# An attention and two-MLP kernel: x2 transposed by VectorE in squares of 32 and placed by DMA, where TensorE and two ScalarE copies did it

## The chip, the cores and the metric

One core of one Trainium2 chip. The time is the device time of one execution in microseconds (us), and the median of several executions is given. Around the profiled execution's span (first to last instruction) lie some 2 us that its time also counts.

## The reference, cut to what matters

```python
def _attn_ref(q, k, v, n_sink, window):            # 2 x 8 heads x 768 x 64
    scores = scale * np.matmul(q, k.transpose(0, 1, 3, 2))
    keep = is_sink | in_window                      # 4 sinks, a window of 128
    a = softmax(np.where(keep, scores, -1e9))
    return np.matmul(a, v)

x = attention, laid out as 1536 tokens x 512
h = x @ w_in                                        # 512 -> 1024
ln = layernorm(h * softmax(h)) * g_ln
x2 = ln @ w_out                                     # 1024 -> 512
g = np.maximum(x2 @ w2_in, 0.0) ** 2                # 512 -> 2048
out = g @ w2_out                                    # 2048 -> 512
```

## The kernel before, in words

The 1536 tokens are worked as NT = 12 tiles of 128. Tile numbers run from 0 to 11. Products are in fp32r: each operand is split into a rounded part (`_hi`) and a rest (`_lo`), and each product is three matmuls.

**Stage A** makes attention, h, the gated layer norm and x2 for one tile after another, as a pipeline that is written out by hand for each engine. `step(t)` (one function of this name on TensorE, ScalarE and VectorE) does at the same time: the values and `hidden` (h) of tile n = t + 1, the transposes of the normalised hidden row `u` and the second projection (`project`, into `x2_ps`) of tile t, and the scores and softmax of tile t + 2. `first_step` and `second_step` are steps 0 and 1; then come steps 2 to 10, the last without scores. Each engine runs its list in order, and semaphores tie the lists together, so where an instruction stands in a list decides what waits behind it.

**x2 before the change.** The matmuls of `project(t, ...)` (L1240) leave x2 of tile t as 128 tokens x 512 in the PSUM bank `x2_ps`, which is the bank `w1_ps` (rows of the trace say `w_ps`). Stage B needs it transposed, with the 512 features on the partitions. So

- ScalarE's `copy_x2` (L622) copies it to the SBUF tile `x2` (rows say `x`), first thing in the next step;
- TensorE's `transpose_x2(t - 1)` (L1268) transposes four blocks of 128x128 into `o_ps`, between `transpose_p(t + 2, 0)` and `transpose_p(t + 2, 1)`, near the end of the step;
- ScalarE's `copy_x2T` (L626) copies `o_ps` into columns t*128 to t*128+127 of `x2T`, a [128, 4, 1536] tile.

`transpose_ln(t)` (L1230) may not overwrite `w1_ps` until `copy_x2(t - 1)` is done, and `values(n, 0)` may not write `o_ps` until `copy_x2T` of tile n - 3 is done.

**VectorE in a step** normalises `u` (`normalize_hidden`, L883, which waits for GpSimd's `rstd`, L444), splits xT and lnT, merges scores and takes the row maxima of tile t + 2 (L827, L839), normalises probabilities in two groups (`normalize_p`, L899 to L904), splits the next K and Q (`split_k` L888, `split_q` L893), takes the maximum of h (`hidden_max`, L844, two halves), and then gates and does the statistics of tile n (`gate_and_norm`, L854 to L871).

**SyncE's queue** issues nearly all DMAs in order. Its loop over n waits for `q_split` and loads Q (L319), waits for `k_split` and loads K (L326), waits for `pv_done` and loads V of tile n - 1 (L331), and for n = 4 to 7 loads a quarter of `w2in` (L378). After the loop it loads the last V, waits for h of tile 11 (`h_done`, 2 * NT) and issues the eight loads of `w2out` (L383).

**Stage B** takes 3 blocks of 512 tokens. `round_x2T(blk)` on ScalarE (L755) and `split_x2T(blk)` on VectorE (L1054) make the two parts of x2T, all four tiles of a block at once; `hidden2` (L1405) and `project2` (L1417) are the products, with `chain` on ScalarE and VectorE in between. The first `hidden2` calls of block 0 are laced with the end of tile 11:

```python
            hidden2(0, 0)
            transpose_x2(NT - 2)
            hidden2(0, 1, 0, 2)
            transpose_ln(NT - 1)
            hidden2(0, 1, 2, 3)
            project(NT - 1, 0, 12).then_inc(wo_half_read, 1)
            project(NT - 1, 12, 24)
            hidden2(0, 1, 3, 4)
            transpose_x2(NT - 1)
```

`project2` writes four banks, one of which is `w1_ps`, so x2 of tile 11 must be out of it before block 0 goes on.

Of the kernel before, what the change touches and what calls it, by code (L numbers as in the profile page):

```python
# [49 lines left out]
BLK = BANK  # L50
NB = T // BLK
# [79 lines left out]
def attention_moe_program(nc, qT, kT, v, w_in, w_out, g_ln, w2_in, w2_out, out):  # L131
# [6 lines left out]
    with ctx:  # L138
# [141 lines left out]
        x2_done, x2T_done = sem("x2_done"), sem("x2T_done")  # L280
# [4 lines left out]
        lnT_split, xT_split, x2T_copied = sem("lnT_split"), sem("xT_split"), sem("x2T_copied")  # L285
# [4 lines left out]
        lnT_rounded, xT_rounded, x2_copied = sem("lnT_rounded"), sem("xT_rounded"), sem("x2_copied")  # L290
# [21 lines left out]
        @block.sync  # L312
        def _(sp):
            def load_q(n):
                if since(n, 3):
                    sp.wait_ge(q_split, n - 2)
                for half in range(2):
                    rows, heads = half_heads(half)
                    sp.dma_start(q_raw[rows, :, :], qT[n, :, heads, :]).then_inc(q_loaded, 16)  # L319

            def load_k(n):
                if since(n, 3):
                    sp.wait_ge(k_split, n - 1)
                for half in range(2):
                    rows, heads = half_heads(half)
                    sp.dma_start(k_raw[rows, :, :], kT[n, :, heads, :]).then_inc(k_loaded, 16)  # L326

            def load_v(n):
                if since(n, 2):
                    sp.wait_ge(pv_done, GROUPS * n)  # L330
                sp.dma_start(V[:, n % 2, :], v[n]).then_inc(v_loaded[n % 2], 16)  # L331

            def load_w_in(c):
                sp.dma_start(w_raw[:, c, :], w_in[c * P:(c + 1) * P, :]).then_inc(w_loaded[c], 16)

            def load_w_out(c):
                sp.dma_start(wo_raw[:, c * C1 // 2:(c + 1) * C1 // 2, :],
                             w_out[c * F1 // 2:(c + 1) * F1 // 2, :].rearrange("(k p) m -> p k m", p=P)
                             ).then_inc(wo_loaded[c], 16)

            def load_k01(n):
                for half in range(2):
                    rows, heads = half_heads(half)
                    sp.dma_start(k01[rows, n, :, :], kT[n, :, heads, :]).then_inc(k01_loaded[n], 16)

            def load_v_sink(b):
                sp.dma_start(v_sink_raw[0:SKS, b, :],
                             v[b * TPB, 0:N_SINK, :].unsqueeze(0).to_broadcast([SPLITS * H, N_SINK, DM])
                             ).then_inc(v_sink_loaded[b], 16)

            load_k01(0)
            load_w_in(0)
            load_w_in(1)
            load_v(0)
            load_k01(1)
            for half in range(2):
                load_q01(sp, 1, half)
            load_w_in(2)
            load_v_sink(0)
            load_w_in(3)  # L360
            load_k(2)
            load_q(2)
            load_v(1)
            load_w_out(0)
            load_w_out(1)
            load_v_sink(1)
            for n in range(3, NT):
                load_q(n)
                load_k(n)
                load_v(n - 1)  # L370
                if n == 4:
                    sp.wait_ge(w_split, MC - 1)
                    sp.wait_ge(w_split_pool, 4)
                    sp.wait_ge(wo_split, len(WO_DVE))
                    sp.wait_ge(wo_split_pool, len(WO_POOL))
                if n in range(4, 4 + MC):
                    c = n - 4
                    sp.dma_start(w2in[:, c, :], w2_in[c * P:(c + 1) * P, :]).then_inc(w2in_loaded, 16)  # L378
            load_v(NT - 1)
            sp.wait_ge(h_done, 2 * NT)  # L380
            sp.wait_ge(h_done, 2 * NT)
            for c in range(C2 // 2):
                sp.dma_start(w2out[:, 2 * c:2 * c + 2, :],  # L383
                             w2_out[2 * c * P:(2 * c + 2) * P, :].rearrange("(c p) m -> p c m", p=P)
                             ).then_inc(w2out_loaded[c], 16)
            with sp.Fori(0, NB) as blk:
                for i in range(TB):

                    sp.wait_ge((y_copied_act, y_copied_dve)[i % 2], TB // 2 * blk + (i // 2 + 1))
                    sp.dma_start(out[bass.ds(blk * BLK + i * P, P), :], y[i]).then_inc(y_stored, 16)  # L390
            sp.wait_ge(y_stored, 16 * TB * NB)

# [156 lines left out]
        def _(act):  # L549
# [70 lines left out]
            def copy_x2(t):  # L620
                act.wait_ge(x2_done, t + 1)
                nc.scalar.copy(x2[:, :], x2_ps[:, :]).then_inc(x2_copied, 1)  # L622

            def copy_x2T(t):
                act.wait_ge(x2T_done, t + 1)
                nc.scalar.activation(x2T[:, :, bass.ts(t, P)], o_ps[:, :].rearrange("p (c q) -> p c q", q=P),  # L626
                                     ACT.Copy).then_inc(x2T_copied, 1)

# [8 lines left out]
            def step(t, nxt=True):  # L637
# [3 lines left out]
                copy_x2(t - 1)  # L641
# [16 lines left out]
            def finish(t):  # L658
# [8 lines left out]
                copy_x2T(t - 1)  # L667
# [26 lines left out]
            def second_step():  # L694
# [5 lines left out]
                copy_x2(0)  # L700
# [51 lines left out]
            def round_x2T(blk):  # L752
                cols = slice(blk * BLK, (blk + 1) * BLK)
                act.wait_ge(x2T_copied, TB * (blk + 1))
# [10 lines left out]
            copy_x2T(NT - 3)  # L765
            hidden_exp(NT - 1)
            copy_x2(NT - 2)
            copy_x2T(NT - 2)
# [18 lines left out]
            copy_x2(NT - 1)  # L787
            chain(1, 1)
            copy_x2T(NT - 1)
# [17 lines left out]
        def _(dve):  # L807
# [110 lines left out]

            def split_v_sink(b):
# [12 lines left out]
            def step(t):  # L932

                n = t + 1
                normalize_hidden(t)
# [5 lines left out]
                row_max(t + 2, 0)  # L941
                merge(t + 2, 2)
# [3 lines left out]
                if t + 3 < NT:  # L946
                    split_k(t + 3)
                    split_q(t + 3)
                hidden_max(n, 0)
                hidden_max(n, 1)  # L950
                hidden_max_all(n)
                normalize_p(t + 2, 1)
# [30 lines left out]
            def second_step():  # L983
# [11 lines left out]
                row_max(3, 0)  # L995
                merge(3, 2)
# [65 lines left out]

            normalize_hidden(NT - 2)
# [7 lines left out]
            gate_and_norm(NT - 1)  # L1071
            normalize_hidden(NT - 1)
# [20 lines left out]
            split_w2out(0)  # L1093
            chain(1, 1)
# [17 lines left out]
        def _(pe):  # L1112
# [41 lines left out]
            def values(n, g):  # L1154

                if g == 0:
                    pe.wait_ge(v_loaded[n % 2], 16 * (n // 2) + 16)
                    if since(n, 3):
                        pe.wait_ge(x2T_copied, n - 2)
# [64 lines left out]
            def transpose_ln(t):  # L1224
                if t:
                    pe.wait_ge(x2_copied, t)
# [36 lines left out]
            def transpose_x2(t):  # L1263
                pe.wait_ge(x2_copied, t + 1)
                if t >= NT - 2:
                    pe.wait_ge(x2T_copied, t)
                for c in range(MC):
                    done = nc.tensor.transpose(o_ps[:, c * P:(c + 1) * P], x2[:, c * P:(c + 1) * P], ident[:, :])  # L1268
                done.then_inc(x2T_done, 1)

# [4 lines left out]
            def step(t, nxt=True):  # L1275
# [23 lines left out]
                transpose_x2(t - 1)  # L1299
# [31 lines left out]
            def second_step():  # L1331
# [19 lines left out]
                transpose_x2(0)  # L1351
# [84 lines left out]
            transpose_x2(NT - 2)  # L1436
# [6 lines left out]
            transpose_x2(NT - 1)  # L1443
# [36 lines left out]
```

## Time and profile before

| | before |
|---|---|
| median of 3 runs | 504.12 us (503.33 to 504.96) |
| the profiled execution's own time | 503.94 us |
| its span | 502.1 us |
| TensorE (PE) busy | 489.4 us, 97% |
| weight loads (PEld) busy | 398.0 us, 79% |
| VectorE (DVE) busy | 279.6 us, 56% |
| ScalarE (ACT) busy | 212.7 us, 42% |
| GpSimd (POOL) busy | 99.0 us, 20% |
| chain that ended last, by engine | PE 86%, DVE 11%, ACT 1%, POOL 1% |
| granted TensorE clock | 0.999 of full |

Busy shares are averages over a stage A of some 240 us and a stage B of some 260 us. A matmul's row is longer than its place in the pipeline: the chain of waits gives the pace (0.23 us a matmul of 512 columns), the single rows give 0.39 us.

### The profile page before, as it was taken

The page shows a single profiled execution, that of the slowest core. Times are in us where ns is not written, and L with a number is a line of the kernel's source. Part 1 is how long each engine was busy: PE and PEld are TensorE (multiplying, and loading weights), DVE is VectorE, ACT ScalarE, POOL GpSimd, SP SyncE. Part 2 cuts the span into 40 slices and gives each one's busy share as a digit, 9 for nine tenths or more (in the row PEclk, how much of TensorE's full clock was granted, in tenths as well). Part 3 has the DMA queues.
Part 4 walks back from the last instruction along what each step waited for, and adds up shares of the span by engine and source line. Part 5 has one row for each costly group of instructions (what it writes and reads, how often), then busy time and mean ns, then how long its engine had stood idle before and what let it go on. Part 6 is the DMA issues. An engine that isn't in the chain of part 4 may idle for free.

```text
span 502.1 us, 7242 instructions
## 1 busy us (share of the span) xinstructions
PE 489.4 (97%) x2692; PEld 398.0 (79%) x2692; DVE 279.6 (56%) x501; ACT 212.7 (42%) x556; POOL 99.0 (20%) x138
## 2 busy tenths in 40 slices
PE   8989899999999999999999999999999999999997
PEld 6667778888788888878877888888888888888885
DVE  4999798777878878756696433332222232232232
ACT  4667556656666665624543322421211232221121
POOL 2555051020022112264994000000000000000000
PEclk9999999999999999999999999999999999999999
DMA  8921241241112100008000000020000002000002
GB/s 254 282 66 46 103 144 48 106 147 44 52 35 63 44 22 22 1 4 332 1 0 2 0 0 1 1 84 0 0 0 0 0 0 84 1 0 0 1 0 84
DMA packets 12069, 26.05 MB, mean 52 GB/s; under 512 B 1608, under 2 KB 1608, under 8 KB 11528
## 3 DMA queue, kind: packets, MB, share of 16 engines
q1 hardware_dynamic: 11736, 25.40, 15.6%
q8 instruction: 18, 0.29, 0.2%
q10 hardware_dynamic: 304, 0.27, 0.2%
q14 instruction: 11, 0.09, 0.1%
HBM read 22.52 MB, written 3.15 MB: 51 GB/s over the span
## 4 chain that ended last, share of the span: by engine, by line
PE 86%; DVE 11%; ACT 1%; POOL 1%; issue 1%; DVEq 0%; POOLq 0%; ACTq 0%
PE score_ps L1405 25%; PE h_ps L1417 12%; PE w_ps L1240 11%; PE h_ps L1202 11%; PE wt_ps L1417 6%; PE w_ps L1417 6%; PE o_ps L1172 3%; PE score_ps L1142 2%; PE wt_ps L1150 2%; PE wt_ps L1142 1%; PE h_ps L1230 1%; DVE prob L904 1%; PE o_ps L1268 1%; PE w_ps L1273 1%; PE o_ps L1189 1%; DVE w2out_lo L1059 1%
## 5 line engine op out<-in xcount | busy, mean ns | idle before, releaser
L1405 PE MATMUL score_ps<-x2T_hi,w2in_hi 128*128 (+1 forms) x192 | 74.9, 390 | 0.0
L1405 PE MATMUL score_ps<-x2T_hi,w2in_lo 128*128 (+1 forms) x192 | 74.7, 389 | 0.0
L1405 PE MATMUL score_ps<-x2T_lo,w2in_hi 128*128 (+1 forms) x192 | 74.7, 389 | 0.0
L1076 DVE TENSOR_TENSOR e<-e 128x512 f32<-128x512 f32 x24 | 18.5, 772 | 81.7 <-ACT e L772 81.7
L1076 DVE TENSOR_TENSOR sq<-relu 128x512 f32<-128x512 f32 x24 | 17.5, 728 | 80.5 <-ACT relu L772 80.5
L772 ACT ACTIVATE relu<-score_ps 128x512 f32<-128x512 f32 x24 | 14.3, 598 | 92.1 <-PE score_ps L1405 92.1
L772 ACT ACTIVATE e<-score_ps 128x512 f32<-128x512 f32 x24 | 14.4, 599 | 87.4 <-PE score_ps L1405 87.3
L1405 PEld LDWEIGHTS score_ps<-x2T_hi,w2in_hi 128*128 128x128 f32 x192 | 36.1, 188 | 7.5
L1405 PEld LDWEIGHTS score_ps<-x2T_hi,w2in_lo 128*128 128x128 f32 x192 | 36.0, 188 | 7.4
L1405 PEld LDWEIGHTS score_ps<-x2T_lo,w2in_hi 128*128 128x128 f32 x192 | 36.0, 188 | 7.4
L582 ACT ACTIVATE prob<-sm,nbias 128x132 f32<-128x132 f32 (+1 forms) x96 | 37.8, 396 | 0.5
L1240 PE MATMUL w_ps<-wo_hi,lnT_hi 128*128 128x512 f32 x88 | 35.5, 404 | 2.3 <-DVE lnT_lo L911 2.2
L1202 PE MATMUL h_ps<-w_hi,xT_hi 128*128 128x512 f32 x88 | 35.5, 404 | 0.7 <-DVE xT_lo L916 0.7
L1240 PE MATMUL w_ps<-wo_lo,lnT_hi 128*128 128x512 f32 x88 | 35.3, 401 | 0.0
L1202 PE MATMUL h_ps<-w_hi,xT_lo 128*128 128x512 f32 x88 | 34.5, 392 | 0.0
L1240 PE MATMUL w_ps<-wo_hi,lnT_lo 128*128 128x512 f32 x88 | 34.4, 390 | 0.0
L1202 PE MATMUL h_ps<-w_lo,xT_hi 128*128 128x512 f32 x88 | 34.3, 390 | 0.0
L544 POOL TENSOR_TENSOR w2in_lo<-w2in,w2in_hi 128x512 fp32r<-128x512 f32 x16 | 25.5, 1597 | 1.3
L601 ACT ACTIVATE e<-h_ps,nhmax 128x512 f32<-128x512 f32 x24 | 16.3, 684 | 18.9 <-DVE nhmax L849 18.8
L425 POOL CAST p_sink<-prob 128x64 fp32r<-128x64 f32 x10 | 2.4, 237 | 110.8 <-DVE prob L904 99.8
L1240 PEld LDWEIGHTS w_ps<-wo_hi,lnT_hi 128*128 128x128 f32 x88 | 16.5, 188 | 7.2 <-DVE lnT_lo L911 3.1
L1202 PEld LDWEIGHTS h_ps<-w_hi,xT_hi 128*128 128x128 f32 x88 | 16.5, 188 | 5.3 <-issue 1.2
(180 smaller groups left out, 1133.5 us busy)
## 6 DMA issues: line engine op xcount, KB each, us to landing
w2in<-w_in SPq DMA_DIRECT2D x4, 1024.0 KB, 4.9
w2out<-w_out SPq DMA_DIRECT2D x8, 512.0 KB, 7.4
V<-v SPq DMA_DIRECT2D x12, 256.0 KB, 2.6
k_raw<-kT SPq DMA_DIRECT2D x20, 132.0 KB, 2.8
q_raw<-qT SPq DMA_DIRECT2D x20, 128.0 KB, 2.8
w2in<-w_in SPq DMA_DIRECT2D x4, 512.0 KB, 6.5
w2in<-w_out SPq DMA_DIRECT2D x2, 1024.0 KB, 11.6
out<-u SPq DMA_DIRECT2D x6, 256.0 KB, 2.0
```

Source lines behind the costliest of these rows:

```text
L544: nc.gpsimd.tensor_tensor(w2in_lo[:, :, fs], w2in[:, :, fs], w2in_hi[:, :, fs].bitcast(F32), ALU.subtract).then_inc(w2in_split, 1)
L582: nc.scalar.activation(prob[:, h, seen(n)], sm[:, h, seen(n)], ACT.Exp, bias=nbias[:, h:h + 1], scale=SCALE, accum_out=psum_row[:, h:h + 1 ...
L601: nc.scalar.activation(e[:, cols], h_ps[:, cols], ACT.Exp, bias=nhmax[:, :], scale=1.0, accum_out=hsum[:, half:half + 1]).then_inc(h_exped, 1)
L772: nc.scalar.activation(relu[f % 2], h2_ps[f % 2], ACT.Relu).then_inc(relu_ready, 1)
L1076: nc.vector.tensor_tensor(sq[f % 2], relu[f % 2], relu[f % 2], ALU.mult).then_inc(sq_ready, 1)
L1142: done = mm(score_banks(n, p)[:, j, cols], qs[rows], ks[rows], start=(n < 2 or i == 0), stop=(n < 2 or i == len(products) - 1))
L1150: last = nc.tensor.transpose(pT_ps[g][:, j * P:(j + 1) * P], prob[:, g * HG + j, main(n)], ident[:, :])
L1172: last = mm(o_ps[rows, cols], V[:, slot, h * D:(h + 1) * D], pT[:, g, j * P:(j + 1) * P], start=(g == 0 and part == 0 and i < 2), stop=(al ...
L1202: done = mm(h_ps[:, cols], xs[:, c, :], ws[:, c, cols], start=(c == 0 and k == 0), stop=(c == MC - 1 and k == 2))
L1240: done = mm(x2_ps[:, :], ls[:, k, :], ws[:, k, :], start=(k == 0 and i == 0), stop=(k == C1 - 1 and i == 2))
L1405: done = mm(h2_ps[f % 2], ws[:, c, fs], xs[:, c, bass.ts(blk, BLK)], start=(c == 0 and i == 0), stop=(c == MC - 1 and i == 2))
L1417: done = mm(y_ps[q], gs[f % 2][:, qs], ws[:, f, :], start=(f == 0 and i == 0), stop=(f == C2 - 1 and i == 2))
```

## The change

VectorE transposes `x2_ps` into `x2` in one instruction, each square of 32x32 in its place. A square then has the right inside and the wrong place: the 16 pairs (token quarter i, feature quarter r) are carried to x2T by 16 DMAs a tile, each of 32 partitions x 4 chunks x 32 elements (128 bytes a run). `transpose_x2`, `copy_x2` and `copy_x2T` and their waits go. On VectorE `split_q` and `normalize_p(t + 2, 1)` also move forward.

```diff
+SQ = 32
+QUADS = P // SQ
+MOVES = 16 * QUADS * QUADS
...
+            def move_x2(t):
+
+                sp.wait_ge(x2_squared, t + 1)
+                squares = x2[:, :].rearrange("p (c r b) -> p c r b", r=QUADS, b=SQ)
+                for i in range(QUADS):
+                    for r in range(QUADS):
+                        sp.dma_start(x2T[r * SQ:(r + 1) * SQ, :, t * P + i * SQ:t * P + (i + 1) * SQ],
+                                     squares[i * SQ:(i + 1) * SQ, :, r, :]).then_inc(x2T_moved[t // TB], 16)
...
             for n in range(3, NT):
+                if n >= 5:
+                    move_x2(n - 5)
                 load_q(n)
                 load_k(n)
                 load_v(n - 1)
...
+            move_x2(NT - 5)
             load_v(NT - 1)
-            sp.wait_ge(h_done, 2 * NT)
+            move_x2(NT - 4)
+            move_x2(NT - 3)
             sp.wait_ge(h_done, 2 * NT)
             for c in range(C2 // 2):
                 sp.dma_start(w2out[:, 2 * c:2 * c + 2, :],
                              w2_out[2 * c * P:(2 * c + 2) * P, :].rearrange("(c p) m -> p c m", p=P)
                              ).then_inc(w2out_loaded[c], 16)
+            move_x2(NT - 2)
+            move_x2(NT - 1)
...
-                copy_x2(t - 1)
...
-                copy_x2T(t - 1)
...
-                act.wait_ge(x2T_copied, TB * (blk + 1))
+                act.wait_ge(x2T_moved[blk], TB * MOVES)
...
-            copy_x2T(NT - 3)
             hidden_exp(NT - 1)
-            copy_x2(NT - 2)
-            copy_x2T(NT - 2)
...
+            def square_x2(t):
+
+                dve.wait_ge(x2_done, t + 1)
+                if t:
+                    dve.wait_ge(x2T_moved[(t - 1) // TB], (t - 1) % TB * MOVES + MOVES)
+                nc.vector.transpose(x2[:, :], x2_ps[:, :]).then_inc(x2_squared, 1)
...
             def step(t):
 
                 n = t + 1
+                square_x2(t - 1)
                 normalize_hidden(t)
...
                 row_max(t + 2, 0)
+                if t + 3 < NT:
+                    split_q(t + 3)
                 merge(t + 2, 2)
                 merge(t + 2, 3)
                 row_max(t + 2, 1)
                 normalize_p(t + 2, 0)
                 if t + 3 < NT:
                     split_k(t + 3)
-                    split_q(t + 3)
                 hidden_max(n, 0)
+                normalize_p(t + 2, 1)
                 hidden_max(n, 1)
                 hidden_max_all(n)
-                normalize_p(t + 2, 1)
                 gate_and_norm(n)
...
+            square_x2(NT - 2)
             normalize_hidden(NT - 1)
...
             chain(0, 0)
             split_w2out(0)
+            square_x2(NT - 1)
             chain(1, 1)
...
-                    if since(n, 3):
-                        pe.wait_ge(x2T_copied, n - 2)
...
                 if t:
-                    pe.wait_ge(x2_copied, t)
+                    pe.wait_ge(x2_squared, t)
...
-                transpose_x2(t - 1)
...
             hidden2(0, 1, 3, 4)
-            transpose_x2(NT - 1)
+            pe.wait_ge(x2_squared, NT)
```

In `second_step` the transpose of tile 0 stands after `row_max(3, 0)`, and that of tile 9 ahead of `normalize_hidden(NT - 2)`.

VectorE, from the row maximum of the first group to the gate in a middle step, before (`nmax` is the row maximum, `QL` the split of Q, `hmax` the two halves of the maximum of h, `prob` the normalised probabilities):

```order
L839 TENSOR_REDUCE nmax<-sm 128x4
L827 COPY_PREDICATED sm<-own_seen,score_ps 128x2x128
L827 COPY_PREDICATED sm<-own_seen,wt_ps 128x2x128
...
L904 TENSOR_TENSOR prob<-prob,rz 128x528
L888 TENSOR_TENSOR KL<-k_raw,KH 128x4x132
L893 TENSOR_TENSOR QL<-q_raw,QH 128x512
L844 TENSOR_REDUCE hmax<-h_ps 128x1 x2
L849 TENSOR_REDUCE nhmax<-hmax 128x1
L899 TENSOR_SCALAR z_eps<-psum_row 128x4
L901 RECIPROCAL rz<-z_eps 128x4
L904 TENSOR_TENSOR prob<-prob,rz 128x528
L854 TENSOR_TENSOR u<-h_ps,e 128x512
```

and now, with the start of the step ahead of it (line numbers of the changed kernel):

```order
L872 TENSOR_TENSOR var<-moments,hz_eps 128x1
L925 STREAM_TRANSPOSE x<-w_ps 128x512
L884 TENSOR_SCALAR u<-u,moments,rstd 128x512 x2
...
L840 TENSOR_REDUCE nmax<-sm 128x4
L894 TENSOR_TENSOR QL<-q_raw,QH 128x512
L828 COPY_PREDICATED sm<-own_seen,score_ps 128x2x128
...
L845 TENSOR_REDUCE hmax<-h_ps 128x1
L900 TENSOR_SCALAR z_eps<-psum_row 128x4
L902 RECIPROCAL rz<-z_eps 128x4
L905 TENSOR_TENSOR prob<-prob,rz 128x528
L845 TENSOR_REDUCE hmax<-h_ps 128x1
L850 TENSOR_REDUCE nhmax<-hmax 128x1
L855 TENSOR_TENSOR u<-h_ps,e 128x512
```

The transpose stands between the variance and the normalisation; QL moved ahead of the second pair of merges, and the second group of probabilities moved between the halves of the maximum of h.

SyncE's queue at the end of stage A, before:

```order
L319 DMA q_raw<-qT 64x512 x2
L326 DMA k_raw<-kT 64x528 x2
L331 DMA V<-v 128x512 x2
L383 DMA w2out<-w_out 128x2x512 x8
```

and now (L342 is the DMA of the moves):

```order
L342 DMA x2T<-x 32x4x32 x16
L322 DMA q_raw<-qT 64x512 x2
L329 DMA k_raw<-kT 64x528 x2
L334 DMA V<-v 128x512
L342 DMA x2T<-x 32x4x32 x16
L334 DMA V<-v 128x512
L342 DMA x2T<-x 32x4x32 x32
L399 DMA w2out<-w_out 128x2x512 x8
L342 DMA x2T<-x 32x4x32 x32
```

Sixteen moves stand ahead of each Q load from tile 5 on, 32 ahead of the w2out loads and 32 behind them.

## Rows read from the trace of the kernel before

**Rows 1.** Chain that ended last, a middle step: start us, us, what.

```profile
156.08 0.44 PE o_ps L1268 x4
...
161.40 0.24 PE w_ps L1230 x2
...
174.11 0.44 PE o_ps L1268 x4
...
175.09 1.83 PE w_ps L1240 x8
```

**Rows 2.** The same chain, second step.

```profile
63.62 1.21 DVE hmax L844 x2
```

**Rows 3.** Timeline of DVE, same middle step: start, us, instruction, [idle before].

```profile
158.94 0.48 DVE L871 TENSOR_TENSOR var<-moments,hz_eps 128x1 f32<-128x1 f32 x1
160.09 1.00 DVE L883 TENSOR_SCALAR u<-u,moments,rstd 128x512 f32<-128x512 f32 x2 [0.68 <-POOL rstd L444]
...
166.50 0.45 DVE L827 COPY_PREDICATED sm<-own_seen,score_ps 128x256 f32<-128x256 uint32 x1 [1.06 <-ACT sm L555]
...
171.67 0.69 DVE L844 TENSOR_REDUCE hmax<-h_ps 128x1 f32<-128x512 f32 x1 [0.46 <-PE h_ps L1202]
...
172.87 0.71 DVE L904 TENSOR_TENSOR prob<-prob,rz 128x528 f32<-128x528 f32 x1
```

**Rows 4.** One line's instructions, L1012: a DVE subtraction of 128x1024.

```profile
L1012 DVE TENSOR_TENSOR w_lo<-w2in,w_hi x3: 1218/1219/1626, 13.2 to 24.1; 128x1024 fp32r<-128x1024 f32 x3
```

**Rows 5.** Timeline of SP's queue: the middle step, then the w2out loads.

```profile
160.85 0.33 SPq L331 DMA_DIRECT2D V<-v  x1
170.64 1.10 SPq L319 DMA_DIRECT2D q_raw<-qT  x2
...
224.57 4.76 SPq L383 DMA_DIRECT2D w2out<-w_out  x8
```

**Rows 6.** One line's DMAs, L319 and L347: issue ns min/median/max, landing us.

```profile
L319 SPq DMA_DIRECT2D q_raw<-qT x20: 465/597/603, 9.5 to 171.1; - x20
...
DMA to landing us min/median/max: 2.5/2.8/8.5
```

```profile
L347 SPq DMA_DIRECT2D v_sink_raw<-v x2: 945/1226/1508, 6.8 to 12.4; - x2
```

**Rows 7.** Timeline of ACT: the middle step, then step 10.

```profile
159.43 0.63 ACT L573 ACTIVATE QH<-q_raw 128x512 fp32r<-128x512 f32 x1
```

```profile
226.99 0.60 ACT L626 ACTIVATE x2T<-o_ps 128x512 f32<-128x512 f32 x1 [8.12 <-PE o_ps L1268]
227.49 0.68 ACT L601 ACTIVATE e<-h_ps,nhmax 128x512 f32<-128x512 f32 x1
```

**Rows 8.** DMA queues: packets, MB, share of 16 engines; DMA issues with landing.

```profile
q1 hardware_dynamic: 11736, 25.40, 15.6%
...
q10 hardware_dynamic: 304, 0.27, 0.2%
...
out<-u SPq DMA_DIRECT2D x6, 256.0 KB, 2.0
...
x2T<-qT ACTq DMA_DIRECT2D x2, 128.0 KB, 4.0
...
g_col<-g_ln ACTq DMA_DIRECT2D x1, 4.0 KB, 5.5
```

**Rows 9.** Chain that ended last, end of stage A.

```profile
241.07 0.65 PE o_ps L1268 x4
241.72 0.69 PE wt_ps L1417 x3
```

**Rows 10.** Timeline of DVE, statistics of tile 11.

```profile
224.51 0.69 DVE L844 TENSOR_REDUCE hmax<-h_ps 128x1 f32<-128x512 f32 x1 [2.03 <-PE h_ps L1202]
...
231.52 0.16 DVE L871 TENSOR_TENSOR var<-moments,hz_eps 128x1 f32<-128x1 f32 x1
```

**Rows 11.** Busy time by stretch; the last two numbers are DMA share and GB/s.

```profile
236.00:238.00 2.00, 2.00 (x11) 1.65 (x10) 1.97 (x2) 0.29 (x1) 1.96 (x2) 1.00 0.77 299
```

More of the change, by code:

```diff
@@ L279, in attention_moe_program @@
         o_done, h_done, lnT_done = sem("o_done"), sem("h_done"), sem("lnT_done")
-        x2_done, x2T_done = sem("x2_done"), sem("x2T_done")
+        x2_done = sem("x2_done")
         maxed, biased, hmax_part, hmax_ready = sem("maxed"), sem("biased"), sem("hmax_part"), sem("hmax_ready")
@@ L284, in attention_moe_program @@
         z_ready, rz_ready, p_normed = sem("z_ready"), sem("rz_ready"), sem("p_normed")
-        lnT_split, xT_split, x2T_copied = sem("lnT_split"), sem("xT_split"), sem("x2T_copied")
+        lnT_split, xT_split, x2T_moved = sem("lnT_split"), sem("xT_split"), [sem(f"x2T_moved{b}") for b in range(NB)]
         w_rounded, w_rounded_act, w_split, wo_rounded, wo_split = sem("w_rounded"), sem("w_rounded_act"), sem("w_split"), sem("wo_rounded"), sem("wo_split")
@@ L289, in attention_moe_program @@
         exped, pT_copied, p_sinkT_copied, h_exped = sem("exped"), sem("pT_copied"), sem("p_sinkT_copied"), sem("h_exped")
-        lnT_rounded, xT_rounded, x2_copied = sem("lnT_rounded"), sem("xT_rounded"), sem("x2_copied")
+        lnT_rounded, xT_rounded, x2_squared = sem("lnT_rounded"), sem("xT_rounded"), sem("x2_squared")
         x2T_rounded, x2T_split = sem("x2T_rounded"), sem("x2T_split")
@@ L618, in round_xT @@
                                      ACT.Copy).then_inc(xT_rounded, 1)
[L620 to L627, printed above, removed]
             def round_w_out(first, last):
@@ L699, in second_step @@
                 round_q(4)
-                copy_x2(0)
                 bias(3, 0)
@@ L786, in _ @@
             round_w2out(0)
-            copy_x2(NT - 1)
             chain(1, 1)
-            copy_x2T(NT - 1)
             for f in range(1, C2):
@@ L995, in second_step @@
                 row_max(3, 0)
+                square_x2(0)
                 merge(3, 2)
@@ L1060, in split_w2out @@
                                         ALU.subtract).then_inc(w2out_split, 1)
+            square_x2(NT - 3)
             normalize_hidden(NT - 2)
@@ L1261, in project_0 @@
                     done.then_inc(x2_done, 1)
[L1263 to L1269, printed above, removed]
             def keep_warm(products):
@@ L1435, in _ @@
             hidden2(0, 0)
-            transpose_x2(NT - 2)
             hidden2(0, 1, 0, 2)
```

1 line of the change is left out of this document (removed).

## The prediction

> **What bounds the kernel now.** I read the page first: TensorE is busy 97% of the span, so only what shortens TensorE's list, or makes it wait, moves the time. Then the chain that ended last. In a middle step every piece of it is TensorE, one right behind the other; the reader should see that the four transposes of x2 stand in it with 0.44 us [rows 1], at 0.11 us each, because they are pipelined. From one set to the next is 174.11 - 156.08 = 18.0 us, the length of a step. In the second step the chain runs through VectorE instead [rows 2], so what TensorE saves there is worth nothing. Third, the timelines of VectorE, ScalarE and SP's queue, to see whether what is added fits in gaps, and last the end of stage A, where tile 11 is handed to stage B.
>
> **What is removed.** TensorE loses 12 sets of transposes. Tile 0's is off the chain: 0. Tiles 1 to 8, in steps 2 to 9: 8 x 0.44 = 3.52. Tile 9, in step 10, and tile 10, inside `hidden2`: 0.44 each. Tile 11's costs 0.65, since it waits for ScalarE's copy [rows 9]. Together 3.52 + 0.88 + 0.65 = 5.05 us. ScalarE's 24 copies (0.60 us each) stand ahead of work that waits for something else, so they are priced at nothing, with one exception: `copy_x2T(9)` holds `hidden_exp(11)` back. The second half of the maximum ends at 225.20 [rows 10] and a small reduction (about 0.2) follows, yet the exp starts at 227.49, behind a copy that waited for TensorE [rows 7]. So the statistics of tile 11 come 2.1 us earlier.
>
> **VectorE's transpose in a middle step.** No row shows this operation. VectorE's work on 512 columns out of PSUM takes 0.69 [rows 3]; an instruction of 1024 columns takes 1.22 [rows 4]. I take 0.70, one pass over as many columns, and keep 1.22 as the upper end. Below 0.69 I see no reason, and it would bring nothing, as the next lines show. It stands after the variance, which ends at 159.42, and ahead of the normalisation, which waits until 160.09 for GpSimd's rstd [rows 3]: 0.67 us idle that just about hold it. Its input, the end of `project`, is there at 158.9 (175.09 + 1.83 a step later shows the same place [rows 1]) and comes 0.44 earlier now. So the transpose ends at 160.16 and the first half of `u` at about 160.7, 0.1 later than before. TensorE asks for it at 161.40 [rows 1], now 0.44 earlier, 160.96. Slack 0.25: cost 0. With 1.22 us it would be 0.27 late, in each of 9 steps: 2.4 us.
>
> **The two moves on VectorE.** QL (0.68) goes into an idle 1.06 us before the third merge [rows 3]: 0. `normalize_p(t + 2, 1)`, 1.1 us, fills the 0.46 idle before the second half of `hmax` and the room that QL left; I place that half at 171.8 for 171.67, and the gate, which stood behind the same `normalize_p` until that ended at 173.58 [rows 3], no longer does. The chain to the variance keeps its time: 0. The probabilities come 1.7 us earlier, so TensorE can close the gap that the x2 transposes leave.
>
> **SP's queue in a middle step.** 16 DMAs of 16 KB a tile. Back to back, a Q load takes 0.60 us to issue [rows 6], the eight w2out loads 4.76 / 8 = 0.595 [rows 5], with four to eight times the bytes. The dearest issues are the v_sink loads, 0.945 and 1.508 [rows 6], whose two sides have different shapes (24 x 4 rows on 96 partitions). The moves have the same shape on both sides, so I take 0.60, near the many rows, and keep 0.33 (the V load, [rows 5]) and 1.51 as ends. The moves start behind the V load, 160.85 + 0.33 = 161.2, and end at 170.8; the Q load was issued at 170.64 [rows 5]. Nothing is late: it lands 2.8 us later [rows 6], and ScalarE's `round_q` comes at 159.43 + 17.57 = 177.0 [rows 7]. In numbers: the second Q load has landed 1.42 + 0.33 + 16c + 0.6 + 2.8 = 5.15 + 16c after the `round_q` before it, c being the issue cost; that must be under 17.57, so c may be 0.77. Next behind Q stand K and V with several us of slack. The wait of `square_x2(t)` for tile t - 1's moves is met 4 us ahead. Cost 0.
>
> **Packets.** A move is 128 runs of 128 bytes, 8 for each of 16 engines, and one semaphore write for each: 144 packets an engine and tile. Queue q1's mean packet takes 15.6% x 16 x 502.1 / 11736 = 107 ns at 2.2 KB [rows 8]: upper end, 15.4 us a tile. On ACT's queue q10 there are 304 packets in about 16 us: 128 of 2 KB, 128 of 32 bytes, 48 for semaphores; with the large ones at 107 ns the small ones are left 14 ns, and 36 ns if the rounded share is 0.25% [rows 8]. I take 14 to 36, 2.0 to 5.2 us a tile, less than the 9.6 us that issuing takes. The Trainium skill (DMA: Bandwidth & Descriptors, Specifications) says that a transfer under 512 bytes is a read-modify-write and misses line rate; it gives no price for 128 bytes, and no row here shows a read-modify-write; by it the sum would move towards the upper end, 512.7 (third rival below), where by the rows of q10 it stays at -2.5.
>
> **The end of stage A** is where a new wait appears. Times are those of before, less the 3.52 us gained by then. h of tile 11 is done at 224.5 - 3.5 = 221.0. SP has finished tile 9's moves at 220.3 (transpose done at 210.6, and 9.6 us), so the w2out loads go out at 221.0 to 225.8 and drain at about 234.3 (before, the stretch to 238 still moved 299 GB/s [rows 11]). The variance of tile 11 ends at 231.68 [rows 10] - 3.52 - 2.11 = 226.05, the transpose of tile 10 at 226.75, its moves are issued until 226.8 + 9.6 = 236.4 and land 2.0 us later (the shortest landing [rows 8]), at 238.4. Only then may VectorE transpose tile 11, though x2 is there at 236.0: done at 239.15. TensorE has nothing left from 241.07 - 4.40 = 236.67 [rows 9] and resumes at 239.2, where it resumed at 241.72 [rows 9]. So 2.5 us of the 5.05 are given back: -5.05 + 2.5 = -2.5 us. Behind the waiting transpose on VectorE stands `chain(1, 1)`, whose result TensorE wants only 5 us after it resumes. After that stage B is as before, earlier by 2.5.
>
> **The sum.** 503.94 (the profiled execution, 0.18 under the median) - 2.5 = 501.4 us.
>
> **Rivals.**
> - *The end gives all back.* With 53 ns a packet, behind w2out's drain at 234.3, tile 10 lands at 241.9, TensorE resumes at 242.7, +1.0: 505. The transpose at 1.22 us also ends here: -2.5 + 2.4 + 0.5, 504. For it: moves queue behind 4 MB in the same rings. Against: q10's small packets look cheap. 0.22.
> - *Slower: SP's queue becomes the bound of a step.* It decides at c = 0.77 for the steps and near 0.73 for the end. At 0.945 a step lasts 5.15 + 15.1 = 20.3, +2.7 for each of the 7 Q loads with moves ahead, 19 us; at the end tile 9's moves hold w2out and tile 10's hold TensorE, +9.3: 503.9 - 2.5 + 19 + 9.3 = 530. At 1.508 it would be 610. For it: the v_sink rows. Against: more than 60 issues at 0.6 or under. 0.17.
> - *Slower: the packets, or a fixed cost of each DMA.* At 107 ns, tile 10 lands at 249.7, TensorE resumes at 250.5, +8.8: 512.7, and Q loads land behind 15.4 us of packets and start to hold ScalarE. If DMAs did not overlap at all, 16 of the shortest landing, 2.0 [rows 8], would take 32 us against a step of 17.6, and `square_x2` would wait 14 us in each of 9 steps: 630. Against: two Q loads issued 0.6 apart each land 2.8 after their own issue [rows 6]. 0.11. The Trainium skill (DMA: Bandwidth & Descriptors, Anatomy of one DMA) fits 2.0 us + bytes / 436e3 to one DMA on the software path; added up that is an estimate of 33 us a tile, as in this rival; overlapped, it is only the landing. The trace speaks for overlap.
> - *Better: no wait at the end* (issue at 0.33 to 0.4 once the rings are free, quick packets): -5.0, 498.9. 0.10, within "faster".
>
> That the change does less than it says I give nothing; the order of the instructions shows it.
>
> **How the numbers follow.** A difference under 0.3% (1.5 us) can't be told from none here. The forecast, -2.5 us with the wait at the end anywhere from 1 to 3.5, has 0.40; with the better case faster has 0.50, same 0.22, slower 0.28. The forecast's own range is 498.9 to 502.5. To leave out no more than 0.2 the range runs to 512, which holds the cases of the end and the milder packet case and leaves SP's queue out. Predicted 501.4.
>
> **What would show it.** No L1268; steps of 17.6 us; STREAM_TRANSPOSE of 0.7; issue of a move 0.6, with Q loads out at the same place; TensorE idle some 2.5 us before the first `project2`, released by the transpose of tile 11, itself by the moves of tile 10. Wrong if ScalarE waits for `q_raw`, if the transpose waits for moves in middle steps, or if steps stay at 18.0.

## The result and the profile after

| | before | after |
|---|---|---|
| median | 504.10 us (503.06 to 505.89, 20 runs) | 505.47 us (503.79 to 506.53, 20 runs) |
| the profiled execution's own time | 503.94 us | 503.79 us |
| its span | 502.1 us | 502.1 us |
| TensorE, VectorE, ScalarE busy | 489.4, 279.6, 212.7 us | 484.4, 287.0, 201.1 us |
| granted TensorE clock | 0.999 in the profiled execution | 0.992 to 0.997 in 19 executions, 1.000 in the profiled one alone |

The ratio is 1.0027, with a 95% interval of 1.0019 to 1.0034: 1.4 us slower, where 2.5 us less was forecast. That is under the 0.3% which the prediction took as no difference; 20 runs of each do resolve it, and it isn't faster. TensorE and ScalarE did lose their work. The profiled execution of the changed kernel is the fastest of its 20 and the only one whose clock stayed at 1.000, so its profile shows only part of the loss. The kernel before was timed 57 times more beside the experiments: its clock was 0.999 or 1.000 in 56 of them and 0.997 in one.

The page of the changed kernel, its engines, its first DMA queue, the chain by engine and the moves:

```profile
PE 484.4 (96%) x2644; PEld 393.3 (78%) x2644; DVE 287.0 (57%) x513; ACT 201.1 (40%) x532; POOL 95.5 (19%) x138
...
q1 hardware_dynamic: 39384, 28.56, 19.6%
...
PE 76%; DVE 14%; SPq 5%; ACT 2%; issue 2%; POOL 1%; DMA 0%; DVEq 0%; POOLq 0%; ACTq 0%
...
x2T<-x SPq DMA_DIRECT2D x192, 16.0 KB, 1.8
```

SP's queue, which is nowhere in the chain before, now has 5% of it. Queue q1 carries 27,648 packets more than in [rows 8] for 4.0 points more of its share: 0.040 x 16 x 502.1 / 27648 = 11.6 ns each. The two new operations, each line's instructions, with ns min/median/max and first to last start:

```profile
L925 DVE STREAM_TRANSPOSE x<-w_ps x12: 702/710/718, 56.1 to 240.0; 128x512 f32<-128x512 f32 x12
```

```profile
L342 SPq DMA_DIRECT2D x2T<-x x192: 585/601/1606, 56.9 to 250.4; - x192
...
DMA to landing us min/median/max: 1.8/1.8/8.6
```

Both prices were right (0.70 and 0.60). The same step as [rows 1], in the chain:

```profile
160.04 0.24 PE w_ps L1242 x2
...
177.62 0.24 PE w_ps L1242 x2
```

A step is 17.6 us here, as forecast. The Q load goes out at 170.88, where it went out at 170.64 before [rows 5], though by then TensorE is 1.36 us ahead of before (160.04 for 161.40 [rows 1]):

```profile
159.87 10.97 SPq L342 DMA_DIRECT2D x2T<-x  x16
170.88 1.24 SPq L322 DMA_DIRECT2D q_raw<-qT  x2
...
195.03 27.13 SPq L342 DMA_DIRECT2D x2T<-x  x32
222.21 5.51 SPq L399 DMA_DIRECT2D w2out<-w_out  x8
```

The end of stage A is where it goes wrong. The chain there, from the first move of tile 10 to stage B's first `project2` (compare [rows 9]; the 13 moves left out are issues of 0.60 to 0.76 with a gap of 0.04 behind each, and the row `DMA x2T<-x` is the 16th move, from the start of its issue to its landing):

```profile
227.77 0.82 SPq L342
228.59 0.04 issue
...
237.20 0.60 SPq L342
...
237.85 2.05 DMA x2T<-x
...
239.99 0.73 DVE x L925
240.72 0.32 issue
241.04 0.96 PE wt_ps L1419 x3
242.00 0.69 PE w_ps L1419 x3
242.69 1.36 PE h_ps L1419 x6
```

And the timelines of VectorE and TensorE, with the idle time ahead of a row in brackets:

```profile
226.96 0.72 DVE L925 STREAM_TRANSPOSE x<-w_ps 128x512 f32<-128x512 f32 x1
...
239.99 0.72 DVE L925 STREAM_TRANSPOSE x<-w_ps 128x512 f32<-128x512 f32 x1 [4.06 <-DMA x2T<-x]
```

```profile
237.12 0.39 PE L1407 MATMUL score_ps<-x2T_hi,w2in_lo 128*128 128x512 f32 x1
241.04 0.49 PE L1419 MATMUL wt_ps<-w2out_hi,g_hi 128*128 128x512 f32 x1 [3.53 <-DVE x L925]
```

The wait is the one foretold: tile 10's squares are in `x2` until its 16 moves have landed, so VectorE can't transpose tile 11 into it, and TensorE stands for 3.53 us. It resumes at 241.04, only 0.68 us ahead of before, and that rest goes in block 0, where TensorE waits 1.29 us for `w2out_lo` at 259.03; before it had two such waits in this block, 0.37 at 258.45 and 0.28 at 269.91, together 0.65.

### The profile page after: what moved, and what is told of

It reads as the page before. It is cut to its first block, busy times and chain, and to the rows that moved or that the text cites. A ratio compares the mean times of both kernels' runs of the same rounds, so it can differ in the third digit from the quotient of the medians.

```text
span 502.1 us, 7334 instructions
## 1 busy us (share of the span) xinstructions
PE 484.4 (96%) x2644; PEld 393.3 (78%) x2644; DVE 287.0 (57%) x513; ACT 201.1 (40%) x532; POOL 95.5 (19%) x138
## 4 chain that ended last, share of the span: by engine, by line
PE 76%; DVE 14%; SPq 5%; ACT 2%; issue 2%; POOL 1%; DMA 0%; DVEq 0%; POOLq 0%; ACTq 0%
PE score_ps L1407 24%; PE h_ps L1419 12%; PE h_ps L1214 9%; PE w_ps L1252 7%; PE wt_ps L1419 6%; PE w_ps L1419 6%; SPq L342 4%; PE o_ps L1184 2%; PE score_ps L1156 2%; PE wt_ps L1164 1%; DVE prob L905 1%; PE wt_ps L1156 1%; DVE bstat L862 1%; SPq L399 1%; DVE u L855 1%
## 5 line engine op out<-in xcount | busy, mean ns | idle before, releaser
L1089 DVE TENSOR_TENSOR sq<-relu 128x512 f32<-128x512 f32 x24 | 18.6, 775 | 83.2 <-ACT relu L775 83.2
L619 ACT ACTIVATE e<-h_ps,nhmax 128x512 f32<-128x512 f32 x24 | 16.3, 684 | 26.6 <-DVE nhmax L850 26.5
L562 POOL TENSOR_TENSOR w2in_lo<-w2in,w2in_hi 128x512 fp32r<-128x512 f32 x16 | 24.1, 1509 | 1.3
L855 DVE TENSOR_TENSOR u<-h_ps,e 128x512 f32<-128x512 f32 x24 | 16.3, 682 | 7.6 <-ACT e L619 7.6
```

The source lines that it names most:

```text
L562: nc.gpsimd.tensor_tensor(w2in_lo[:, :, fs], w2in[:, :, fs], w2in_hi[:, :, fs].bitcast(F32), ALU.subtract).then_inc(w2in_split, 1)
L619: nc.scalar.activation(e[:, cols], h_ps[:, cols], ACT.Exp, bias=nhmax[:, :], scale=1.0, accum_out=hsum[:, half:half + 1]).then_inc(h_exped, 1)
L855: nc.vector.tensor_tensor(u[:, cols], h_ps[:, cols], e[:, cols], ALU.mult).then_inc(u_ready, 1)
L1089: nc.vector.tensor_tensor(sq[f % 2], relu[f % 2], relu[f % 2], ALU.mult).then_inc(sq_ready, 1)
```

## The theories and the experiments

The other 19 executions were slower than the profiled one by 0.7 to 2.7 us at a lower clock. **Theory A**: the wait at the end costs twice: TensorE's idle time, and a fall of its clock that follows from it. **Theory B**: the wait only takes what the trace shows; the rest is variation from 192 more DMAs. **Theory C**: block 0 is bound by something else there, so that what is gained ahead of it is swallowed whatever the wait. Before's medians for the three sets of runs are 504.12 (e0 to e3), 504.11 (e4, e5, e7, e8) and 504.45 us (e6, e9, e10).

**e0_after**, the changed kernel again, to see its usual execution.

> The changed kernel once more, for its clock. Theory A (the wait at the end of stage A costs twice: TensorE idles 3.7 us before the first project2, and in most executions its granted clock then falls to its lower level for some us): the profile shows either a clock of 1.00 and 502 us of span, or stretches below 1.00 right behind the idle 3.7 us and 503 to 504.5 us of span; median 505.4. Theory B (the small DMAs vary from execution to execution, and Q loads or the moves of tile 10 land later): a slower execution shows clock dips elsewhere or longer waits for q_raw and for the moves, with the end of the idle stretch 1 to 2 us later than 241.0.

Measured: 505.62 us (504.86 to 507.71, 12 runs), ratio 1.0021 (1.0004 to 1.0039), clock 0.992 to 0.997 in all 12. This time the profile fell on such an execution. TensorE's timeline, then the stretches around the wait (columns: length, then PE, PEld, DVE, ACT and POOL busy, PEclk, DMA share, GB/s), then the chain:

```profile
241.64 0.49 PE L1419 MATMUL wt_ps<-w2out_hi,g_hi 128*128 128x512 f32 x1 [3.81 <-DVE x L925]
...
243.59 0.63 PE L1419 MATMUL h_ps<-w2out_hi,g_hi 128*128 128x512 f32 x1
```

```profile
240.00:242.00 2.00, 0.36 (x2) 0.32 (x3) 1.41 (x2) 0.00 (x0) 1.92 (x3) 1.00 0.01 4
242.00:244.00 2.00, 2.00 (x7) 1.53 (x6) 1.97 (x3) 0.00 (x0) 1.92 (x2) 0.64 0.14 22
244.00:246.00 2.00, 2.00 (x6) 1.59 (x5) 1.14 (x1) 0.00 (x0) 1.92 (x3) 0.50 0.17 26
246.00:248.00 2.00, 2.00 (x10) 1.64 (x10) 0.00 (x0) 0.00 (x0) 1.92 (x3) 1.00 0.16 25
```

```profile
242.60 1.19 PE w_ps L1419 x3
243.79 2.45 PE h_ps L1419 x6
```

After an idle of 3.8 us the granted clock is 0.64 and 0.50 of full in two stretches, that is at its 1.2 GHz level for the greater part of the first and all of the second, and then full again. The fall shows only after TensorE has started again: its first matmuls, those that start up to 242.44, still take 0.39 to 0.51 us, those from 242.74 on take 0.63. Nine matmuls took 1.19 + 2.45 = 3.64 us where the first trace has 0.69 + 1.36 = 2.05: 1.6 us lost. The Trainium skill (TensorE: Matmul & The Clock Gate, Part 1) calls the throttled clock the default, which activity lifts; by that rule, a wait of TensorE is not over when it ends, and this trace agrees.

**e1_spare**, one edit: tile 11 is transposed into a spare tile, `y[3]`, so there is nothing to wait for. All 192 moves stay.

```diff
-                if t:
+                if t and t < NT - 1:
                     dve.wait_ge(x2T_moved[(t - 1) // TB], (t - 1) % TB * MOVES + MOVES)
-                nc.vector.transpose(x2[:, :], x2_ps[:, :]).then_inc(x2_squared, 1)
+                nc.vector.transpose(y[3] if t == NT - 1 else x2[:, :], x2_ps[:, :]).then_inc(x2_squared, 1)
...
-                squares = x2[:, :].rearrange("p (c r b) -> p c r b", r=QUADS, b=SQ)
+                squares = (y[3] if t == NT - 1 else x2[:, :]).rearrange("p (c r b) -> p c r b", r=QUADS, b=SQ)
```

> Tile 11 is transposed into another buffer (y[3], free by then), so VectorE need not wait for tile 10's moves. Theory A: TensorE resumes at about 237.8 instead of 241.04 (the transpose follows x2_done at 236.9), the clock stays at 1.00 in every execution, and the median is 500.5 to 502.5, or 503.8 if block 0 swallows the 3.2 us. Theory B: the median falls by no more than 3.2 us less what varies, with the clock still 0.992 to 0.997. Theory C (in block 0 VectorE is the bound while GpSimd still splits w2in, so what TensorE gains before it is lost in it): TensorE resumes at 237.8 but the profiled span stays at 502 give or take 0.5, and VectorE's late w2out_lo holds project2 longer than the 1.3 us seen now.

Measured: 499.79 us (499.35 to 501.31, 6 runs), ratio 0.9912 (0.989 to 0.9933), clock 0.999 to 1.000. TensorE's timeline:

```profile
238.30 0.49 PE L1419 MATMUL wt_ps<-w2out_hi,g_hi 128*128 128x512 f32 x1 [0.41 <-DVE y L925]
```

3.1 us of idle time are gone, block 0's wait is 0.55 us instead of 1.29, and the kernel is 4.3 us faster than before and 5.8 faster than e0. The gain reaches the end, so C falls, but for what block 0 took in the first trace. With every DMA kept, the clock stays up.

**e2_warm** keeps the wait and fills most of it: 16 matmuls that nobody reads go into a free bank.

```diff
             hidden2(0, 1, 3, 4)
+            for _ in range(16):
+                mm(w0_ps, w2in_hi[:, 0, 0:P], x2T_hi[:, 0, 0:BLK], start=True, stop=True)
             pe.wait_ge(x2_squared, NT)
```

> Sixteen matmuls of 512 columns (3.6 us) into a bank that the next project2 starts afresh fill the idle stretch; the wait itself stays. Theory A: TensorE resumes at 241.0 to 241.3 as before, the clock is 1.00 in every execution, median 503.7 to 504.2, 1.3 to 1.7 under the changed kernel. Theory B: median 505.4, no change.

Measured: 503.74 us (502.94 to 506.81, 12 runs), ratio 0.999 (0.9974 to 1.0007), clock 0.999 or 1.000 in 11 of 12. Same wait, same DMAs, work added, and 505.62 - 503.74 = 1.9 us faster than e0: that is the clock's share, and B falls. Its trace shows VectorE still waiting for the moves, and TensorE busy up to 0.20 us before it goes on:

```profile
242.16 0.72 DVE L925 STREAM_TRANSPOSE x<-w_ps 128x512 f32<-128x512 f32 x1 [4.35 <-DMA x2T<-x]
```

```profile
243.21 0.49 PE L1419 MATMUL wt_ps<-w2out_hi,g_hi 128*128 128x512 f32 x1 [0.20 <-issue]
```

The wait without the clock is 503.74 - 499.79 = 3.95 us. The traces of e2 and e1 account for it: from the transposes of `u` of tile 11 to the first `project2` there are 243.21 - 231.52 = 11.69 us in e2 and 238.30 - 230.03 = 8.27 in e1, 3.4 more, and block 0's wait is 1.15 us for 0.55, 0.6 more.

**e3_onemove** carries each tile with one DMA of 128 partitions instead of 16. x2T gets the wrong elements.

```diff
-MOVES = 16 * QUADS * QUADS
+MOVES = 16
...
-                for i in range(QUADS):
...
+                sp.dma_start(x2T[:, :, t * P:(t + 1) * P], x2[:, :].rearrange("p (c q) -> p c q", q=P)).then_inc(x2T_moved[t // TB], 16)
```

> One DMA of 128 partitions a tile (the whole of x2, untransposed as to its squares, so x2T holds wrong places) instead of 16; everything else as in the change. It separates TensorE's gain from what 16 DMAs cost SP's queue. If Q loads are what lost 0.9 of the 3.5 us in the steps, h of tile 11 is done at 221.0 instead of 221.9; the wait at the end goes (TensorE resumes at 237 to 237.8) and the clock stays 1.00. Then 499 to 501.5 by theory A, 502 of span by theory C.

Measured: 499.82 us (499.46 to 501.67, 6 runs), as e1. TensorE resumes at 237.90 after 0.41 us. ScalarE doesn't wait for `q_raw` at all here; in e1 and in the changed kernel it does:

```profile
ACT QH L591 <- DMA q_raw<-qT: 7.4, 6, 3.4
```

These 7.4 us in 6 waits (line of the changed kernel: total, times, longest; 6.2 in 4 in e1) cost nothing that can be measured, since e3 is no faster than e1: the 16 DMAs cost time only through the wait at the end.

**e4_reorder** is the kernel before with VectorE's new order alone (`split_q` and the second `normalize_p` moved forward in `step`, as in the diff of the change).

```diff
                 row_max(t + 2, 0)
+                if t + 3 < NT:
+                    split_q(t + 3)
...
                     split_k(t + 3)
-                    split_q(t + 3)
                 hidden_max(n, 0)
+                normalize_p(t + 2, 1)
                 hidden_max(n, 1)
                 hidden_max_all(n)
-                normalize_p(t + 2, 1)
```

> The kernel before with nothing but VectorE's new order in the steps (the split of Q and the second group of probabilities moved forward). Theory A' (the gain is TensorE's 12 sets of transposes, the order only makes room): 504.1 give or take 0.5. Theory D (part of the gain of the spare buffer kernel, 4.3 us, is the order's): 502.5 to 503.5, since hidden_max would sooner release the exp and the gate.

Measured: 504.28 us (503.49 to 506.08, 12 runs), ratio 1.0004 (0.9993 to 1.0015): nothing that the times show.

**e5_old_order** is e1 with VectorE's old order.

```diff
                 row_max(t + 2, 0)
-                if t + 3 < NT:
-                    split_q(t + 3)
                 merge(t + 2, 2)
...
                     split_k(t + 3)
+                    split_q(t + 3)
                 hidden_max(n, 0)
-                normalize_p(t + 2, 1)
                 hidden_max(n, 1)
                 hidden_max_all(n)
+                normalize_p(t + 2, 1)
```

> The spare-buffer kernel with VectorE's old order. Theory A': with the split of Q late, transpose_p(t + 2, 1) on TensorE, which has lost the x2 transposes that stood before it, waits for the probabilities that end at 173.58 in the old order (old times), while TensorE would ask at 174.11: nothing; 499.8 to 500.3. Theory D: the old order gives back 1 us or more: 500.8 to 503.

Measured: 498.97 us (498.58 to 499.33, 4 runs), ratio 0.9899 (0.9885 to 0.9914). 0.8 us faster than e1. The intervals of the two ratios overlap, but the slowest of these four runs (499.33) lies just under the fastest of e1's six (499.35). The traces say where the time goes, in step 5. The chain of e1 there:

```profile
134.70 0.71 DVE prob L905
135.41 0.62 DVE hmax L845
...
136.05 0.17 DVE nhmax L850
...
141.22 0.72 DVE x L925
...
141.94 0.56 DVE u L884
142.50 0.14 issue
142.63 0.41 PE w_ps L1242 x2
```

and the same place of e5's:

```profile
140.57 0.60 PE o_ps L1200 x4
141.16 0.24 PE w_ps L1241 x2
```

In e1 TensorE waits for `u` there:

```profile
142.63 0.41 PE L1242 MATMUL w_ps<-ident,u 128*128 128x128 f32 x2 [0.43 <-DVE u L884]
```

Behind that stand the `normalize_p` that moved forward, the second half of `hmax` after it, and VectorE's transpose. In e5 TensorE has no such wait, and its chain stays on TensorE. e3, whose ScalarE doesn't wait for Q, has the same 17.63 us in this step as e1, so it isn't the Q load. From the start of the transposes of `u` in one step to the next, TensorE takes 142.63 - 125.00 = 17.63 us in e1 and 141.00 - 123.92 = 17.08 in e5 (17.62 in the changed kernel, 17.48 before; e4, the new order without the transpose, 17.64): 0.55 us. The rest of the 0.8 is not placed; profiled executions differ by as much ahead of all edits (the transposes of `u` of tile 0 start at 38.37 in e1 and 37.31 in e5).

**e7_early_q** is e1 with `split_q(4)` moved forward in `second_step` as well, ahead of the first `square_x2`.

```diff
                 row_max(3, 0)
+                split_q(4)
                 square_x2(0)
...
                 split_k(4)
-                split_q(4)
```

> The spare-buffer kernel, with the split of Q of tile 4 also moved forward in second_step, into the 2.1 us in which VectorE is idle there. The chain runs through VectorE from 60.3 to 72.2 us in the second step, and this takes 0.6 us of it away: median 499.2, 0.6 under the spare-buffer kernel. If the Q load of tile 5 (ScalarE waited 3.4 us for it) is what sets the start of step 2 instead, no change: 499.8.

Measured: 499.53 us (498.39 to 500.79, 6 runs), ratio 0.991 (0.9896 to 0.9925). The trace gains 0.6 in that step (TensorE's transposes of `u` start 71.23 - 58.38 = 12.85 us after those of the step ahead; 13.45 in e1); the times can't tell that from nothing.

**e8_no_pe** is the kernel before without TensorE's 12 sets of x2 transposes, with VectorE's and SyncE's lists kept: ScalarE's second copy takes x2 as it stands, so x2T isn't transposed and that copy no longer waits for TensorE. (ScalarE's part of the edit is left out here.)

```diff
                 pe.wait_ge(x2_copied, t + 1)
-                if t >= NT - 2:
-                    pe.wait_ge(x2T_copied, t)
-                for c in range(MC):
-                    done = nc.tensor.transpose(o_ps[:, c * P:(c + 1) * P], x2[:, c * P:(c + 1) * P], ident[:, :])
-                done.then_inc(x2T_done, 1)
```

> The kernel before without TensorE's transposes of x2 alone (ScalarE copies x2 untransposed into x2T, all other instructions and waits stay). It prices the 12 sets by themselves. By the sum of the prediction 5.05 us: 499.1. If the chain's 0.44 us a set is right but the second term, the last set, is mostly the wait for ScalarE's copy, which stays: 499.6. By the busy time of single rows (0.27 us each, 13 us in all): 491. If other waits take their place, as at the end of stage A: 501 to 503.

Measured: 499.33 us (498.89 to 499.82, 4 runs), ratio 0.9904 (0.989 to 0.9918). The sets, with the waits that go with them, are worth 4.8 us; 5.05 were counted.

**e6_double** is e1 with each move cut in two along the chunks: 32 DMAs a tile, the same bytes and runs.

```diff
-MOVES = 16 * QUADS * QUADS
+MOVES = 2 * 16 * QUADS * QUADS
...
+                        for half in (slice(0, 2), slice(2, MC)):
+                            sp.dma_start(x2T[r * SQ:(r + 1) * SQ, half, t * P + i * SQ:t * P + (i + 1) * SQ],
+                                         squares[i * SQ:(i + 1) * SQ, half, r, :]).then_inc(x2T_moved[t // TB], 16)
```

> The spare-buffer kernel with each move cut in two (2 chunks of features each): 32 DMAs a tile, the same bytes. It tests the rule that the slower rival stands on: a step can't be shorter than 5.15 us + the time that SP takes to issue a tile's moves. At the 0.64 to 0.68 us a DMA that the changed kernel shows, 32 take 20.5 to 21.8 us, so a step would last 25.6 to 27.0 instead of 17.6 where a Q load stands behind the moves, 7 times, +56 to +66, and tile 9's and 10's moves hold w2out and TensorE by some 20 more: 565 to 590. If issue time goes by bytes or by runs rather than by DMA (0.32 us each), no change: 500.

Measured: 589.9 us (589.54 and 590.25), ratio 1.1668 (1.1618 to 1.1718). SP's queue and what ScalarE waited for (total, times, longest):

```profile
81.62 21.76 SPq L343 DMA_DIRECT2D x2T<-x  x32
103.43 1.23 SPq L322 DMA_DIRECT2D q_raw<-qT  x2
...
107.09 21.41 SPq L343 DMA_DIRECT2D x2T<-x  x32
128.54 1.23 SPq L322 DMA_DIRECT2D q_raw<-qT  x2
```

```profile
ACT QH L592 <- DMA q_raw<-qT: 66.5, 7, 13.6
```

A DMA half as large still takes 0.6 us to issue, so issuing is paid by the DMA and not by the byte, and the Q loads are now 25.1 us apart. The rule of the second rival, a step of 5.15 + 16c once c passes 0.77, gives 5.15 + 21.4 = 26.6 with the 21.41 us of 32 moves in the place of 16c, 1.5 us too long. What the trace shows is another bound: the queue never pauses, and 25.1 us is the sum of its own issues, 21.4 for the moves and 3.7 for Q, K, V and `w2in`. The changed kernel stood under that, with 10.97 of a step's 17.6 us for its moves. What holds TensorE here is `u`, behind VectorE's transpose, which waits for the moves of the tile before:

```profile
PE w_ps L1243 <- DVE u L885: 48.9, 10, 8.9
```

```profile
DVE x L926 <- DMA x2T<-x: 51.4, 10, 8.9
```

So the lengthening is not ScalarE's wait for Q alone, as the rival had it. The mean granted clock is 0.924 here and 1.000 in e1, so the clock has a part in it too.

**e10_half_warm** is e2 with 8 filler matmuls, which leave an idle of 2.4 us.

```diff
+            for _ in range(8):
```

> The changed kernel with 8 filler matmuls (1.8 us) instead of 16, so TensorE idles some 1.9 us ahead of the first project2. If the clock falls only after a longer idle stretch: clock 1.00, median 503.7. If any idle of about 2 us brings it down: 505.4 with a clock of 0.992 to 0.997.

Measured: 504.90 us (502.68 to 505.77, 12 runs). The times fall in two groups: five executions at a clock of 1.000 took 502.68 to 503.87 us, seven at 0.995 to 0.997 took 504.88 to 505.77. TensorE's timeline of one of the five:

```profile
237.17 1.97 PE L1445 MATMUL wt_ps<-x2T_hi,w2in_hi 128*128 128x512 f32 x8
241.57 0.49 PE L1419 MATMUL wt_ps<-w2out_hi,g_hi 128*128 128x512 f32 x1 [2.43 <-DVE x L925]
```

The clock fell in 7 of 12 executions here, in 31 of 32 of the changed kernel and e0, and in 1 of 12 of e2; the idle stretches of their profiled executions are 2.4 us, 3.5 and 3.8, and 0.2. Within one kernel the two groups lie some 1.5 us apart, which is the clock's price by another way.

**e9_best** joins what helped: the spare tile, the old order in `step`, and the early `split_q(4)` (the edits of e1, e5 and e7).

> Spare buffer, VectorE's old order in the steps, and the early split of Q in second_step only. If both effects hold and add: 498.97 less 0.3 to 0.6, so 498.4 to 498.7. If the early split alone brings nothing: 499.0.

Measured: 498.37 us (497.73 to 499.0, 6 runs), ratio 0.986 (0.9834 to 0.9886). It beats the kernel before by 6.1 us and the changed one by about 7. In its trace that place of step 5 takes 17.05 us and that of `second_step` 12.85, so both effects are there together.

## Why the prediction was wrong

The mechanism was foretold, its size was not. By medians, from 504.1: the x2 transposes -4.8 (e8; e5 with everything but the wait and the new order -5.1), VectorE's new order +0.8 (e1 against e5), the wait +3.95 (e2 against e1), the clock +1.9 (e0 against e2). From e5's -5.1 the sum is +1.5 us. That sum is no test by itself, since its terms are the steps from e5 by e1 and e2 to e0, and it must end at e0's own difference; what stands apart from it is the first result, +1.4, and e8, whose -4.8 agrees with e5's -5.1. Against the prediction the clock is 1.9 us that had no term, the wait is 3.95 for 2.5, and the new order 0.8 for 0.

- **What is removed**: right. 4.8 for 5.05.
- **VectorE's transpose in a middle step**: right. 0.71 us, in the gap ahead of `rstd`, no wait in steps 6 to 9. In the second step it stands in the chain ahead of `u`, and the time from the step ahead is the same as before (72.32 - 58.88 = 13.44, before 72.14 - 58.69 = 13.45).
- **The two moves on VectorE**: wrong, by the steps that were not looked at. "The chain to the variance keeps its time: 0" was argued on one middle step. In step 5 VectorE has less room (before, it ran the two halves of `hmax` there back to back, from 134.85, where the middle step has 0.46 us idle between them), and the later `hmax` together with the transpose holds TensorE: 0.55 us in the trace, 0.8 by the medians. Alone on the kernel before, the order costs nothing that the times show (e4).
- **SP's queue in a middle step**: right in price (0.60, with gaps of 0.04 that were not counted) and in result. The price was read from loads with 8 and 32 times a move's bytes (128 and 512 KB for 16), not four to eight, which speaks for it the more. ScalarE does wait for `q_raw`, which the prediction named as a sign against it, but those waits cost nothing (e3). The edge of 0.77 for c wasn't tested: e6 went past another, the sum of the queue's own issues.
- **Packets**: 11.6 ns, under the low end of 14 to 36. The read-modify-write that the Trainium skill (DMA: Bandwidth & Descriptors, Specifications) states doesn't show as a price here: 27,648 packets fit in 4 points of the queue's share. And a landing of 1.8 us with issues 0.64 apart shows the overlap that the third rival denied.
- **The end of stage A**: this is the step that failed, with the term below that is missing in it. Foretold was a TensorE that runs dry at 236.67, idles 2.5 us and resumes at 239.2; it ran dry at 237.51, idled 3.53 and resumed at 241.04. The 1.84 us are four terms in a row. The moves started at 227.77 instead of 226.8 (0.97). The queue did not do that: tile 9's moves kept the w2out loads until 222.21 and they ended at 227.72, but VectorE's transpose of tile 10 itself ended only at 227.68, and in e3, where the queue is free, the first move goes out at 227.68 as well. The transpose was late because h of tile 11 came 2.61 us earlier than before (221.90 for 224.51 [rows 10]) and not 3.52. Of the 0.91 us that are missing, step 5 had lost 0.58 (17.62 for 17.48 less 0.44), the other sets gave 0.39 to 0.44 each (0.16 in all), and 0.18 is the start of this execution. The foretold 2.1 us for the statistics were right (2.06). Next, issuing took 0.48 more, and by luck no more than that: 15 issues took 10.08 us, where 9.0 was their price, but the prediction counted a 16th, 0.60, ahead of a landing which is measured from the start of that issue. Landing took 2.05 (0.05), and VectorE and TensorE each took a moment to start (0.34, with the 0.02 of the longer transpose). Of the 1.84 us, 0.84 is that all of TensorE's work was later by then; 1.0 is a longer wait. Block 0 then took 0.64 more than before (1.29 for 0.65), where "stage B is as before" was foretold; in e1, without the wait, it is 0.55. What moves it there was not traced.
- **The missing term**: the clock. The prediction had TensorE idle for 2.5 us and priced that at 2.5. No term, no bound and no rival had what the clock does after an idle, although the kernel itself has a function, `keep_warm`, with which TensorE issues matmuls that nobody reads, at its start and in its first step. It cost 1.9 us, and with the actual idle it came in 31 of 32 executions. The foretold 2.5 us of idle would not have been safe either: with 2.4 the clock fell in 7 of 12 (e10).

Of the rivals, *the end gives all back* had the right sign and size (504 to 505) for a wrong reason, so its number is luck: packets were not slow and the transpose took 0.71; the late transpose of tile 10, issuing and the clock made the time.

## What to carry to other kernels

Where a change frees TensorE in each step but puts a transfer between two uses of one buffer, look at the last use: what hides the transfer in the steps is gone there, and one more buffer (e1) was worth 5.8 us, more than all that the change takes from TensorE (4.8). An idle of TensorE has to be priced twice, as its length and as what the clock costs after it; here 3.95 and 1.9 us. And an instruction order must be checked in the tightest step, not in a typical one.

## What was not expected of the hardware

- The clock fell to the 1.2 GHz level after an idle of 3.5 to 3.8 us in 31 of 32 executions, and after one of 2.4 us in 7 of 12, in the same place of the same program; its price was 1.5 to 1.9 us. (The idle was read in one profiled execution of each kernel.) In 12 of the 32 the mean was 0.992 or 0.993, over twice the loss of the profiled 0.997. No profile fell on one of these, so whether there the clock stays low for longer or falls a second time is open; their median is 505.69 us for 505.44 of the other 19, so little of it reached the time.
- SP's queue takes some 0.6 us and a gap of 0.04 to issue a DMA of 8 KB (0.597 in the median, e6), 16 KB (0.601) or 128 KB (0.597 before), and no longer for 512 KB (0.546), and 16 of the moves in a row keep it for 10.97 us in the step shown and 10.25 in one of e5's, even where each lands 1.8 us after its issue starts.
- 128-byte runs between parts of SBUF cost 11.6 ns a packet, semaphore writes among them.
